# High and low part of a norm factor in different rows of one operand, spread by one matmul

## The chip, the cores and the metric

The kernel runs on one core of one Trainium2 chip. The metric is the device time of one execution in microseconds (us), lower is better.

## The reference

```python
kv  = einsum('bhsd,bhse->bhde', k, v)          # 8 batches, 8 heads, 576 tokens, 64 features
out = einsum('bhsd,bhde->bhse', q, kv)
rms = sqrt(mean(out * out, axis=-1, keepdims=True) + 1e-06)
x   = out / rms * g_norm                        # one factor 1/rms for each token and head
x   = x.transpose(0, 2, 1, 3).reshape(4608, 512)
x   = (sigmoid(x @ w_gate) * (x @ w_val)) @ w_mid      # 512 -> 1536 -> 512
h   = x @ w_in                                          # 512 -> 2048
out = where(h > 0, h, exp(min(h, 0)) - 1) @ w_out       # 2048 -> 512
```

All arrays are float32.

## The kernel before

Attention comes first (to about 178 us of the span), then the four large products, which take the rest. The large products use seven sub-products for each 2 by 2 block product, and split each operand into a high and a low part in a reduced float32 format (`F32R`), so that one product is three matmuls.

Attention works on pairs of heads: 8 batches of 4 pairs, 32 pairs in all. Each engine runs its own program, written out by hand, in the same numbered steps; only semaphores tie the engines together. In PE's step p (the code calls its place in a group of eight `r`):

- valid(0): six transposes of q of pair p (L825), then twelve matmuls k'v of pair p (L832), which wait until the kv copies of pair p-1 are out of PSUM
- valid(LO), LO = 1: q times kv of pair p-1, features in rows, tokens in columns, in two halves c = 0, 1 of 288 tokens (L841)
- valid(LB), LB = 7: "spread": the norm factors of pair p-7 are copied to the 64 feature rows of each head (L850 with the high part of the factor, L851 with the low part, for each half c), into PSUM `RB[c]`
- valid(LM), LM = 2: the sums of squares of pair p-2, again as high and low part, added into one PSUM bank `MS` over a whole batch of four pairs (L863, L865). For pair m and half c, head h, the sum lands in row 2(4c + m) + h, so 16 of the 128 rows hold something

After the last pair of a batch (steps with r = 1 or 5) ACT takes the root of all of `MS` (L1042, `rms`) and DVE takes the reciprocal (L1326, `rinv`). In the following step (r = 2 or 6) ACT rounds `rinv` to `r_hi` (L1026), and GpSimd (POOL) computes `r_lo = rinv - r_hi` (L794). PE's spread of the first pair of that batch stands in the step after (r = 3 or 7); it waits on `s_rlo` before its first matmul. I call the steps r = 1, 2, 3 (5, 6, 7) with this hand-over the batch boundary; it comes eight times, with the spreads of PE's steps 7, 11, 15, 19, 23, 27, 31 and 35.

The order on the other engines within a step is what this case turns on:

- DVE: copy kv of the step's pair from PSUM (L1310); `low_squares` for half 0 (L422); the two multiplies of `o` by the spread factor for pair p-7 (L1318); `copy_q` for two pairs ahead (L1301); in steps r = 1 and 5 the reciprocal (L1326)
- ACT: copies of the transposed q (L1019); in steps r = 2 and 6 `r_hi` (L1026); for each half `o` out of PSUM (L1034) and its square rounded (L1036); `copy_k` (L1009); in steps r = 1 and 5 `rms` (L1042)
- POOL: in steps r = 2 and 6 `r_lo` (L794); the squares of both halves (L802); `low_squares` for half 1 (L422)
- SP issues the loads of q, k, v three pairs ahead and the store of each finished pair

PE's spread of half c waits, beside `s_rlo`, for the multiply that read `RB[c]` last.

PE's steps from 32 on stand between the first sub-products of the gated product (L903); there DVE and ACT also split the first activations and form their sums (`sum_x`, L1358 to L1366), and POOL's `weight_sums` (L782 to L788) follows its last attention step. Constants are made by POOL at the start: `sum_f` holds 1/64 in the column of each head, `spread_f` a one in row 2n + h for the 64 columns of head h of factor row n; ACT and DVE wait for the count CONSTANTS.

Of the kernel before, what the change touches and what calls it, by code (L numbers as in the profile page):

```python
# [5 lines left out]
ALU = mybir.AluOpType  # L6
# [16 lines left out]
def build(  # L23
# [98 lines left out]
    with ctx:  # L122
# [23 lines left out]
        ident = ctx.enter_context(nc.sbuf_tensor("ident", [SP_, SP_], F32))  # L146

        with ExitStack() as stack:
            (qkv, sq, sq_hi, sq_lo, rinv, r_hi, r_lo, sum_w, spread_w, o, qt, kv, rms, raw_w, tmp_w, out_w, sum_f, spread_f,
             qk) = view(stack, [  # L150
                 ("qkv", [SP_, QR, 3, 2, RT, D], F32, 12 * KIB),
                 ("sq", [P, 2, HN], F32, 69 * KIB),
                 ("sq_hi", [P, 2, 2, HN], F32R, 69 * KIB + 2304),
                 ("sq_lo", [P, 2, 2, HN], F32R, 69 * KIB + 6912),
                 ("rinv", [P, HN], F32, 69 * KIB + 11520),
                 ("r_hi", [P, 2, HN], F32R, 69 * KIB + 12672),
                 ("r_lo", [P, 2, HN], F32R, 69 * KIB + 14976),
                 ("sum_w", [P, H, P + 2], F32R, 69 * KIB + 17280),
                 ("spread_w", [P, H, 2, D], F32R, 69 * KIB + 21440),
                 ("o", [P, RING, S], F32, buf_at(0)),  # L160
                 ("qt", [P, 2, S], F32, buf_at(0) + RING * S * 4),
                 ("kv", [P, 2, P], F32, buf_at(0) + (RING + 2) * S * 4),
                 ("rms", [P, HN], F32, buf_at(0) + (RING + 2) * S * 4 + KIB),
                 ("raw_w", [P, 2, 2048], F32, buf_at(1)),
                 ("tmp_w", [P, 2, 512], F32, buf_at(1) + 16 * KIB),
                 ("out_w", [P, 2, 2, 512], F32R, buf_at(1) + 20 * KIB),
                 ("sum_f", [P, H, P + 2], F32, buf_at(2)),
                 ("spread_f", [P, H, 2, D], F32, buf_at(2) + 4160),
                 ("qk", [SP_, QK, 2, RT, 2, D], F32, buf_at(3)),
             ])  # L170
# [257 lines left out]
        def ends_batch(r):  # L428
            return (r - LM) % NP == NP - 1
# [318 lines left out]
                sp.wait_ge(s_st[c], 16 * UNITS)  # L748


        IDENTITY, CONSTANTS = 2, 9

        @block.gpsimd
        def _(pool):
# [10 lines left out]
            pool.wait_ge(s_const, 6)  # L765

            for h in range(2):
                pool.memset(sum_f[h * D:(h + 1) * D, :, h:h + 1], 1.0 / D).then_inc(s_const, 1)
                pool.wait_ge(s_const, 7 + h)

            pool.affine_select(out=spread_f[:, :, :, :], in_=spread_f[:, :, :, :], compare_op=ALU.not_equal, fill=1.0,
                               base=0, pattern=[[-2, H], [-1, 2], [0, D]], channel_multiplier=1).then_inc(s_const, 1)
            pool.wait_ge(s_const, CONSTANTS)

            def weight_sums(c):

# [11 lines left out]
                pool.tensor_tensor(b21, b21, t2, ALU.subtract).then_inc(s_wsum, 1)  # L788

            def step(trip, r, valid):  # L790
                if valid(LM + 1) and ends_batch(r - 1):
                    b = batch_of(trip, r - LM - 1)
                    pool.wait_ge(s_rhi, b + 1)
                    pool.tensor_tensor(r_lo[:, batch_of(0, r - LM - 1) % 2, :], rinv[:, :], r_hi[:, batch_of(0, r - LM - 1) % 2, :].bitcast(F32),  # L794
                                       ALU.subtract).then_inc(s_rlo, 1)
                if valid(LO):
                    n = trip * RING + r - LO
                    for c in range(2):
                        pool.wait_ge(s_o_sb, 2 * n + c + 1)
                        wait_count(pool, s_sqlo[c], n)  # L800
                        src = o[:, (r - LO) % RING, half(c)]
                        pool.tensor_tensor(sq[:, c, :], src, src, ALU.mult).then_inc(s_sq, 1)  # L802
                    low_squares(pool, trip, r, 1)
# [10 lines left out]
        def _(pe):  # L814
            pe.wait_ge(s_const, IDENTITY)

            def step(trip, r, valid):
# [25 lines left out]
                if valid(LB):  # L843
                    n = p - LB
                    pe.wait_ge(s_rlo, batch_of(trip, r - LB) + 1)
                    for c in range(2):
                        wait_count(pe, s_x, 2 * n + c - 1)
                        w = spread_w[:, factor_rows(r - LB, c)].rearrange("p h d -> p (h d)")
                        b2 = batch_of(0, r - LB) % 2
                        pe.matmul(RB[c][:, 0:HN], w, r_hi[:, b2, :], start=True, stop=False)  # L850
                        pe.matmul(RB[c][:, 0:HN], w, r_lo[:, b2, :], start=False, stop=True).then_inc(s_rb, 1)  # L851
                if valid(LM):
                    n = p - LM
                    m = (r - LM) % NP
# [151 lines left out]
        def _(act):  # L1006
# [4 lines left out]
            def step(trip, r, valid, ahead=True):  # L1011
# [10 lines left out]
                if valid(LM + 1) and ends_batch(r - 1):  # L1022
                    b = batch_of(trip, r - LM - 1)
                    act.wait_ge(s_rinv, b + 1)
                    wait_count(act, s_rb, 2 * NP * (b - 1))
                    act.activation(r_hi[:, batch_of(0, r - LM - 1) % 2, :], rinv[:, :], ACT.Copy).then_inc(s_rhi, 1)  # L1026
                if valid(LO):
                    n = p - LO
                    if not isinstance(p, int) or n >= RING:
# [268 lines left out]
        def _(dve):  # L1298
# [4 lines left out]
            def step(trip, r, valid, ahead=True):  # L1303
# [15 lines left out]
                                                 op0=ALU.mult, op1=ALU.mult).then_inc(s_x, 1)  # L1319
                if ahead:  # L1320
                    copy_q(trip, r + LC)
                if valid(LM) and ends_batch(r):
                    b = batch_of(trip, r - LM)
                    dve.wait_ge(s_rms, b + 1)
# [282 lines left out]
```

## Time and profile before

| | |
|---|---|
| median of 3 runs | 1717.75 us (1716.82 to 1718.13) |
| profiled execution | 1718.92 us, its span 1716.8 us, 2.1 us outside the span |
| instructions | 27282 |
| TensorE matmul (PE) busy | 1652.0 us, 96% of the span |
| DVE, ACT, POOL busy | 1203.9 us, 839.5 us, 180.4 us |
| mean granted TensorE clock | 0.992 |
| chain that ended last | PE 72%, DVE 6%, ACT 5%, DMA 3% |

The span runs from the first to the last instruction. Matmuls are pipelined: the duration of one includes its way through the array, so what one more matmul costs in a row of them is the distance between starts, not the duration.

### The profile page before, as it was taken

What the parts mean: (1) busy time and instruction counts of PE and PEld (TensorE: products, weight loads), DVE (VectorE), ACT (ScalarE), POOL (GpSimd) and SP (SyncE); (2) the same over time, 40 slices, a digit from 0 to 9 for tenths busy, and PEclk for the clock granted to TensorE, in tenths of its full rate; (3) what the DMA queues carried; (4) which work ended last, traced back from release to release, by engine and by line L of the source; (5) the groups of instructions that cost most, each with busy time, mean ns of one, the idle gap of its engine ahead of it and who ended that gap; (6) DMA issues with size and microseconds to landing.
All of it is one profiled execution on the core that took longest, in us unless ns stands there. A gap on an engine that the chain in (4) does not pass through costs nothing.

```text
span 1716.8 us, 27282 instructions
## 1 busy us (share of the span) xinstructions
PE 1652.0 (96%) x10536; PEld 1628.6 (95%) x10536; DVE 1203.9 (70%) x1429; ACT 839.5 (49%) x1283; POOL 180.4 (11%) x185
## 2 busy tenths in 40 slices
PE   6998899999999999999999999999999799999999
PEld 5887899999999999999999989999999799999999
DVE  5778788887588755777777666776764667677664
ACT  6776455554455544444444444554453444444443
POOL 4555122221022100000000000000000000000000
PEclk9999899999999999999999999999999999999999
DMA  9885488887878645554444664323328833333341
GB/s 263 234 275 175 149 302 297 307 301 258 297 284 300 239 152 212 193 214 167 147 147 148 242 236 148 138 102 139 138 111 327 313 123 124 126 123 124 127 143 60
DMA packets 194745, 339.34 MB, mean 198 GB/s; under 512 B 13376, under 2 KB 149568, under 8 KB 194624
## 3 DMA queue, kind: packets, MB, share of 16 engines
q1 hardware_dynamic: 194624, 337.69, 56.2%
q8 instruction: 80, 1.31, 0.3%
q14 instruction: 41, 0.34, 0.1%
HBM read 191.89 MB, written 145.75 MB: 197 GB/s over the span
## 4 chain that ended last, share of the span: by engine, by line
PE 72%; DVE 6%; ACT 5%; issue 4%; DMA 3%; SPq 1%; POOL 0%; ACTq 0%; DVEq 0%; POOLq 0%
PE pair L903 36%; PE pair L968 21%; PE pair L936 15%; DVE s L1405 3%; DVE e L1510 2%; DMA u_elu<-s 1%; ACT e L1198 1%; DMA weight_items<-out_w 1%; DMA weight_items<-out_x 1%; ACT s L1217 1%; ACT e L1234 1%; ACT e L1229 1%; SPq L518 1%; DMA wreg<-weight_items 1%; ACT s L1208 0%
## 5 line engine op out<-in xcount | busy, mean ns | idle before, releaser
L903 PE MATMUL pair<-ring,wreg 128*128 128x384 f32 x5040 | 888.3, 336 | 29.5 <-ACT s L1217 15.3
L903 PEld LDWEIGHTS pair<-ring,wreg 128*128 128x128 f32 x5040 | 878.2, 189 | 38.5 <-ACT s L1217 20.7
L968 PE MATMUL pair<-wreg,ring 128*128 128x256 f32 x3024 | 364.9, 284 | 6.8 <-DMA wreg<-weight_items 6.8
L968 PEld LDWEIGHTS pair<-wreg,ring 128*128 128x128 f32 x3024 | 364.7, 193 | 7.0 <-DMA wreg<-weight_items 7.0
L1405 DVE TENSOR_TENSOR s<-s,pair 128x768 f32<-128x768 f32 (+1 forms) x252 | 210.5, 835 | 174.6 <-PE pair L903 139.4
L936 PE MATMUL pair<-ring,wreg 128*128 128x384 f32 x1512 | 262.2, 334 | 0.0
L936 PEld LDWEIGHTS pair<-ring,wreg 128*128 128x128 f32 x1512 | 262.1, 188 | 0.0
L1329 DVE TENSOR_TENSOR ring<-raw,ring 128x1024 fp32r<-128x1024 f32 (+1 forms) x162 | 180.7, 1133 | 112.5 <-ACT ring L1104 97.5
L1198 ACT ACTIVATE e<-e 128x768 f32<-128x768 f32 x72 | 61.0, 847 | 186.1 <-DVE e L1510 186.1
L1104 ACT ACTIVATE ring<-raw 128x1024 fp32r<-128x1024 f32 x108 | 111.8, 1051 | 55.9 <-DVE raw L1363 41.3
L1329 DVE TENSOR_TENSOR ring<-sum,ring 128x768 fp32r<-128x768 f32 (+1 forms) x90 | 91.8, 1031 | 30.3 <-ACT ring L1104 13.5
L1514 DVE SCALAR_TENSOR_TENSOR s<-e,s 128x768 f32<-128x768 f32 x72 | 69.0, 958 | 44.8 <-ACT e L1198 43.8
L1428 DVE TENSOR_TENSOR ub<-s 128x384 f32<-128x384 f32 x108 | 67.5, 625 | 12.4 <-ACT s L1125 5.3
L1329 DVE TENSOR_TENSOR ring<-x_raw,ring 128x768 fp32r<-128x768 f32 x72 | 72.0, 1003 | 0.7 <-ACT ring L1073 0.7
L1329 DVE TENSOR_TENSOR ring<-raw_k,ring 128x768 fp32r<-128x768 f32 x54 | 48.7, 953 | 22.6 <-ACT ring L1082 22.3
L1082 ACT ACTIVATE ring<-raw_k 128x768 fp32r<-128x768 f32 x54 | 41.8, 836 | 42.2 <-DVE raw_k L1363 22.6
L832 PE MATMUL pair<-qkv,qk 96*128 96x128 f32 x384 | 52.1, 288 | 2.9 <-DVE kv L1310 2.7
L832 PEld LDWEIGHTS pair<-qkv,qk 96*128 96x128 f32 x384 | 47.9, 200 | 4.4 <-issue 4.1
L1135 ACT ACTIVATE s<-s 128x384 f32<-128x384 f32 x36 | 19.0, 527 | 67.4 <-DVE s L1405 67.4
L1125 ACT ACTIVATE s<-s 128x384 f32<-128x384 f32 x36 | 19.0, 527 | 66.6 <-DVE s L1405 66.6
L1082 ACT ACTIVATE ring<-raw 128x768 fp32r<-128x768 f32 x54 | 41.6, 837 | 19.7 <-PE pair L936 19.7
L422 DVE TENSOR_TENSOR sq_lo<-sq,sq_hi 128x288 fp32r<-128x288 f32 x32 | 27.6, 861 | 30.3 <-POOL sq L802 28.3
(99 smaller groups left out, 1520.3 us busy)
## 6 DMA issues: line engine op xcount, KB each, us to landing
wreg<-weight_items SPq DMA_DIRECT2D x98, 512.0 KB, 6.4
raw<-u_elu SPq DMA_DIRECT2D x36, 1024.0 KB, 7.5
u_gated<-ub SPq DMA_DIRECT2D x144, 192.0 KB, 3.4
u_elu<-s SPq DMA_DIRECT2D x72, 384.0 KB, 2.4
weight_items<-out_w SPq DMA_DIRECT2D x50, 512.0 KB, 4.5
weight_items<-out_x SPq DMA_DIRECT2D x48, 512.0 KB, 4.5
x_raw<-x_attention SPq DMA_DIRECT2D x48, 384.0 KB, 5.5
raw_k<-u_gated SPq DMA_DIRECT2D x6, 2304.0 KB, 8.1
```

The source lines that it names most:

```text
L832: mm = pe.matmul(KV[:, 0:P], qk[:, r % QK, 1, t], qkv[:, r % QR, 2, :, t, :], start=(t == 0), stop=(t == RT - 1))
L903: mm = pe.matmul(dst[:, g, 0:NT], w[:, a, cols], ring[:, slot, b, kt, :], start=(i in STARTS and kt == a == b == 0), stop=(kt == 1 and a = ...
L936: mm = pe.matmul(dst[:, g, 0:NT], w[:, a, cols], ring[:, slot2(vis, i, t), b, kt, :], start=(i in STARTS and t == kt == a == b == 0), stop ...
L968: mm = pe.matmul(dst[:, 0, 0:256], s[:, b, 2 * c + kt, :], w[:, a, cols], start=(i in STARTS and c == kt == a == b == 0), stop=(c == 3 and ...
L1082: act.activation(ring[:, slot2(vis, i, t), 0], mid_item(i, t), ACT.Copy).then_inc(s_hi, 1)
L1104: act.activation(ring4[:, slot4(vis, i), 0], out_item(vis, i), ACT.Copy).then_inc(s_hi, 1)
L1198: act.activation(buf[:, :, :], buf[:, :, :], ACT.Exp).then_inc(s_exp, 1)
L1329: dve.tensor_tensor(dst, src, hi.bitcast(F32), ALU.subtract).then_inc(s_lo, 1)
L1405: dve.tensor_tensor(acc, acc, pp, ALU.add).then_inc(s_comb, 1)
L1428: dve.tensor_tensor(ub[:, m, :], acc[:, 1, :], acc[:, 0, :], ALU.mult).then_inc(s_u, 1)
L1510: dve.tensor_scalar(e[:, :, :], acc[:, :, :], 0.0, None, ALU.min).then_inc(s_min, 1)
L1514: dve.scalar_tensor_tensor(out=acc[:, :, :], in0=e[:, :, :], scalar=-1.0, in1=acc[:, :, :], op0=ALU.add, op1=ALU.max).then_inc(s_e, 1)
```

## The change

The factor's sums are made twice: `sum_f` gets a second column of 1/64 for each head, 64 columns further, so that rows 64 to 79 of `MS` (and of `rms` and `rinv`) repeat rows 0 to 15. `r_hi` and `r_lo` become one tile `r_parts`. ACT rounds all of `rinv` into it, and then rows 64 to 127 are overwritten by `rinv - r_parts`, the low part. `spread_f` gets a second set of ones, 64 rows further down, so that one matmul over 128 rows adds high and low part. The subtraction moves from POOL, where it was the first operation of its step, to DVE, where it stands behind `copy_q`, and has 64 rows instead of 128. POOL makes the constants with two more memsets and one more `affine_select`.

```diff
-                 ("r_hi", [P, 2, HN], F32R, 69 * KIB + 12672),
-                 ("r_lo", [P, 2, HN], F32R, 69 * KIB + 14976),
+                 ("r_parts", [P, 2, HN], F32R, 69 * KIB + 12672),
...
-        IDENTITY, CONSTANTS = 2, 9
+        IDENTITY, CONSTANTS = 2, 12
...
             for h in range(2):
-                pool.memset(sum_f[h * D:(h + 1) * D, :, h:h + 1], 1.0 / D).then_inc(s_const, 1)
-                pool.wait_ge(s_const, 7 + h)
-
-            pool.affine_select(out=spread_f[:, :, :, :], in_=spread_f[:, :, :, :], compare_op=ALU.not_equal, fill=1.0,
-                               base=0, pattern=[[-2, H], [-1, 2], [0, D]], channel_multiplier=1).then_inc(s_const, 1)
-            pool.wait_ge(s_const, CONSTANTS)
+                for at in (h, D + h):
+                    pool.memset(sum_f[h * D:(h + 1) * D, :, at:at + 1], 1.0 / D).then_inc(s_const, 1)
+            pool.wait_ge(s_const, 10)
+
+            for base in (0, -D):
+                pool.affine_select(out=spread_f[:, :, :, :], in_=spread_f[:, :, :, :], compare_op=ALU.not_equal,
+                                   fill=1.0, base=base, pattern=[[-2, H], [-1, 2], [0, D]],
+                                   channel_multiplier=1).then_inc(s_const, 1)
+                pool.wait_ge(s_const, 11 if base == 0 else CONSTANTS)
...
# POOL, step
-                if valid(LM + 1) and ends_batch(r - 1):
-                    b = batch_of(trip, r - LM - 1)
-                    pool.wait_ge(s_rhi, b + 1)
-                    pool.tensor_tensor(r_lo[:, batch_of(0, r - LM - 1) % 2, :], rinv[:, :], r_hi[:, batch_of(0, r - LM - 1) % 2, :].bitcast(F32),
-                                       ALU.subtract).then_inc(s_rlo, 1)
...
# PE, step, valid(LB)
-                        pe.matmul(RB[c][:, 0:HN], w, r_hi[:, b2, :], start=True, stop=False)
-                        pe.matmul(RB[c][:, 0:HN], w, r_lo[:, b2, :], start=False, stop=True).then_inc(s_rb, 1)
+                        pe.matmul(RB[c][:, 0:HN], w, r_parts[:, b2, :], start=True, stop=True).then_inc(s_rb, 1)
...
# ACT, step
-                    act.activation(r_hi[:, batch_of(0, r - LM - 1) % 2, :], rinv[:, :], ACT.Copy).then_inc(s_rhi, 1)
+                    act.activation(r_parts[:, batch_of(0, r - LM - 1) % 2, :], rinv[:, :], ACT.Copy).then_inc(s_rhi, 1)
...
# DVE, step
                 if ahead:
                     copy_q(trip, r + LC)
+                if valid(LM + 1) and ends_batch(r - 1):
+                    dve.wait_ge(s_rhi, batch_of(trip, r - LM - 1) + 1)
+                    low = r_parts[D:P, batch_of(0, r - LM - 1) % 2, :]
+                    dve.tensor_tensor(low, rinv[D:P, :], low.bitcast(F32), ALU.subtract).then_inc(s_rlo, 1)
                 if valid(LM) and ends_batch(r):
```

## Rows read from the trace of the kernel before

**Rows 1.** A stretch: length, busy PE, PEld, DVE, ACT, POOL; PE clock; DMA share, GB/s.

```profile
100.00:120.00 20.00, 19.39 (x148) 17.88 (x147) 15.50 (x33) 16.12 (x36) 12.14 (x16) 1.00 0.89 268
```

**Rows 2.** Groups by line, 0 to 260 us: busy us, mean ns, idle before.

```profile
L851 PE MATMUL pair<-r_lo,spread_w 128*128 128x288 f32 x64 | 18.6, 301 | 0.0
...
L794 POOL TENSOR_TENSOR r_lo<-rinv,r_hi 128x288 fp32r<-128x288 f32 x8 | 6.5, 808 | 30.1 <-ACT r_hi L1026 30.1
...
L771 POOL TENSOR_SCALAR_AFFINE_SELECT spread_f<-spread_f 128x1024 f32<-128x1024 f32 x1 | 1.2, 1167 | 0.1
```

**Rows 3.** Timeline of an ordinary step: start us, us, engine, line, operation.

```profile
85.75 0.66 PE L825 MATMUL pair<-ident,qk 96*128 96x96 f32 x6
...
88.38 0.51 PE L850 MATMUL pair<-r_hi,spread_w 128*128 128x288 f32 x1
...
88.72 0.29 PE L851 MATMUL pair<-r_lo,spread_w 128*128 128x288 f32 x1
...
89.64 0.66 PE L825 MATMUL pair<-ident,qk 96*128 96x96 f32 x6
```

**Rows 4.** Timeline of one batch boundary (PE's steps 21, 22, 23).

```profile
104.87 0.66 PE L825 MATMUL pair<-ident,qk 96*128 96x96 f32 x6
...
110.92 1.94 DVE L1326 RECIPROCAL rinv<-rms 128x288 f32<-128x288 f32 x1
...
112.79 0.41 DVE L1310 COPY kv<-pair 64x64 f32<-64x64 f32 x2
...
113.25 0.39 ACT L1034 ACTIVATE o<-pair 128x288 f32<-128x288 f32 x1
...
114.17 1.29 POOL L802 TENSOR_TENSOR sq<-o 128x288 f32<-128x288 f32 x2
...
114.76 1.14 PE L841 MATMUL pair<-qt,kv 128*128 128x288 f32 x4
114.87 0.91 DVE L422 TENSOR_TENSOR sq_lo<-sq,sq_hi 128x288 fp32r<-128x288 f32 x1 [1.67 <-POOL sq L802]
...
115.81 0.94 DVE L1318 SCALAR_TENSOR_TENSOR o<-o,g_col,pair 128x288 f32<-128x288 f32 x2
...
116.47 0.37 PE L850 MATMUL pair<-r_hi,spread_w 128*128 128x288 f32 x1 [0.58 <-DVE o L1318]
...
116.67 0.55 DVE L1301 COPY qk<-qkv 96x768 f32<-96x768 f32 x1
...
117.14 0.47 DVE L1310 COPY kv<-pair 64x64 f32<-64x64 f32 x2
...
117.71 0.66 PE L825 MATMUL pair<-ident,qk 96*128 96x96 f32 x6
```

**Rows 5.** Line 422 on DVE: ns min/median/max, first and last start.

```profile
L422 DVE TENSOR_TENSOR sq_lo<-sq,sq_hi x32: 479/903/918, 24.8 to 156.8; 128x288 fp32r<-128x288 f32 x32
```

**Rows 6.** Timeline at the first boundary (PE's step 7).

```profile
46.30 0.51 PE L850 MATMUL pair<-r_hi,spread_w 128*128 128x288 f32 x1
46.31 1.16 DVE L1301 COPY qk<-qkv 96x768 f32<-96x768 f32 x1
```

**Rows 7.** Timeline behind PE's step 31 (what PE waited for).

```profile
153.13 2.29 PE L841 MATMUL pair<-qt,kv 128*128 128x288 f32 x4 [1.79 <-DVE kv L1310]
```

**Rows 8.** The stretches before and behind it, columns as in the first group.

```profile
150.00:153.10 3.10, 1.34 (x8) 1.04 (x8) 3.01 (x5) 1.76 (x4) 2.97 (x3) 1.00 0.27 100
153.10:156.40 3.30, 3.27 (x9) 2.69 (x10) 3.26 (x5) 1.65 (x5) 1.59 (x3) 0.51 0.23 89
```

**Rows 9.** Timeline of the last boundary and what follows.

```profile
163.26 0.91 POOL L794 TENSOR_TENSOR r_lo<-rinv,r_hi 128x288 fp32r<-128x288 f32 x1 [4.92 <-ACT r_hi L1026]
...
169.10 4.21 PE L903 MATMUL pair<-ring,wreg 128*128 128x384 f32 x12 [4.09 <-ACT s L1122]
```

**Rows 10.** Line 1366, the sum S4 of the activations: ns min/median/max, first and last start.

```profile
L1366 DVE TENSOR_TENSOR sum<-x_raw,sum x18: 949/951/1950, 164.3 to 1245.1; 128x768 f32<-128x768 f32 x18
```

**Rows 11.** Waits between 45 and 145 us: total us, times, longest.

```profile
ACT qk L1009 <- DMA qkv<-in_k_dram: 7.3, 8, 3.1
```

More of the change, by code:

```diff
@@ L148, in build @@
         with ExitStack() as stack:
-            (qkv, sq, sq_hi, sq_lo, rinv, r_hi, r_lo, sum_w, spread_w, o, qt, kv, rms, raw_w, tmp_w, out_w, sum_f, spread_f,
+            (qkv, sq, sq_hi, sq_lo, rinv, r_parts, sum_w, spread_w, o, qt, kv, rms, raw_w, tmp_w, out_w, sum_f, spread_f,
              qk) = view(stack, [
```

## The prediction

> **What bounds the kernel now.** The change touches attention alone, a tenth of the span, so I read the table of stretches first: at 100 to 120 us PE is busy 19.39 of 20 us, at full clock [rows 1]. PE is the limit in an ordinary step. The groups by line give the size of the target: 64 low-part matmuls, 18.6 us busy [rows 2]. That is not what they cost. In the timeline of an ordinary step the starts run from 88.72 to 89.64 over seven matmuls, so one more costs 0.13 us [rows 3]. The step takes 89.64 - 85.75 = 3.89 us. All 64 would be worth 64 x 0.13 = 8.3 us if PE were the limit everywhere, half a per cent of the kernel.
>
> Then I followed one batch boundary through all engines, as the code's order says it must pass there through DVE [rows 4]. The reader is to see a chain that is not PE's: reciprocal at 110.92, kv copy behind it at 112.79, then PE's k'v matmuls, which need PSUM emptied by that copy, and q times kv at 114.76; and beside it ACT's `o` at 113.25, POOL's squares at 114.17, DVE's `low_squares` at 114.87, its multiplies at 115.81, and PE's spread at 116.47, for which PE stood idle 0.58 us. The reciprocal starts 110.92 - 104.87 = 6.05 us after the first of the three steps began, by way of that step's own `o`, squares and multiplies, and not by way of the spread matmuls. So in the three steps the end is set by DVE's order; only the fourth step of each batch is wholly PE's.
>
> **The change, part by part.**
>
> *Removed on PE.* Two of the four spread matmuls in each step: 0.26 us, so an ordinary step goes from 3.89 to 3.63 us. In the steps r = 1 and 2 this is taken back: PE reaches step r = 3 earlier by 0.52 us and waits that much longer for the kv copy, which still comes at 112.79. So q times kv stays at 114.76.
>
> *Removed on POOL.* `r_lo`, 0.81 us each [rows 2], stood ahead of the squares. Without it these start when `o` is there: 113.25 + 0.39 + 0.08 = 113.72 instead of 114.17, 0.45 us earlier. `low_squares` (114.42), the multiplies (115.36) and `copy_q` (116.22) follow 0.45 us earlier.
>
> *Moved to DVE.* The subtraction now stands behind `copy_q`, whose successor starts 117.14 - 116.67 = 0.47 us after it: 116.22 + 0.46 = 116.68. ACT's `r_hi` stands ahead of the `o` of 113.25 in ACT's order and is long done. PE's spread of this very step waits for the subtraction. What it lasts no row shows; the nearest is the same operation on 128 rows, with 288 elements in each: 0.48 at least, 0.90 median, 0.92 at most [rows 5]. Below 0.48 I see no reason, since what counts is the elements in a row, and halving the rows should do nothing. The long form is the one in which POOL's squares run beside it, and POOL's squares of the next step come up at about that time; I take 0.91 and keep 0.48.
>
> The Trainium skill has the same in "SBUF — State Buffer", section "Who interferes with whom": a VectorE instruction with two SBUF inputs and a GpSimd instruction that reads SBUF exclude each other, and the later one waits for the other's end. By it the subtraction takes 0.48 us or nearly twice that, according to who comes first, and the rows at 0.48 and 0.90 agree.
>
> *The sum at a boundary.* Spread at 116.68 + 0.91 + 0.10 = 117.69 instead of 116.47: +1.22. From there to the next step it took 117.71 - 116.47 = 1.24, of which 0.26 goes with the matmuls and some 0.10 was a wait for the second multiply, now past: 0.88. The next step starts at 118.57, +0.86. The fourth step gives back 0.26. A batch is longer by 0.60 us; with 0.48 for the subtraction by 0.17. What is queued behind the subtraction is the kv copy (117.14, now about 117.6), needed by PE only behind the transposes that start at 118.57, so nothing further is late. There are five such batches (spreads of steps 11 to 27): +3.0 us (0.85 to 3.2).
>
> *First boundary.* Spread at 46.30, without a wait, while `copy_q` starts at 46.31 and takes 1.16 [rows 6]. Now `copy_q` at 45.86, the subtraction behind it at about 47.0 and alone on the port, 0.48, spread at 47.5: +1.2, less 0.4 as above: +0.8.
>
> *Spread of step 31.* There is no `copy_q` any more; the subtraction comes before the first activation sums and the kv copy for which PE waits until 153.13 [rows 7]: about 0.75 us more on DVE less 0.45 from POOL, +0.3, less 0.26 from step 28: +0.05.
>
> *The tail.* After 153.13 PE runs without a wait to the last sums of squares, first at half clock (0.51 [rows 8], so a matmul costs 0.26): two removed at 0.26, two at 0.13: -0.8. Then comes DVE: reciprocal, multiplies, now the subtraction (+0.5), then sum S4, on which ACT's queue and PE's start at 169.10 hang [rows 9]. S4 is the first of its 18 and took 1.95 against 0.95 for the median [rows 10], while POOL ran `weight_sums`, held back to 164.1 by its wait of 4.92 us for `r_hi` [rows 9]. Without that wait POOL is through before S4. That would give back 1.0, but puts POOL beside earlier DVE work; I take -0.3 in all (+0.5 to -0.5). The spread of step 35 lies in PE's wait of 4.09 and gives nothing. The four matmuls removed in steps 36 and 37 lie on the path to the next DVE result: 0.5 to 0.8, taken as -0.6.
>
> *Nothing.* The second `affine_select` (1.17 us [rows 2]) and two small memsets at the start lie under the first loads, for which POOL's weight sums and ACT's and DVE's first copies wait; uncovered they would cost some 1.3 us once. `MS`, `rms`, `rinv` keep their shapes.
>
> Sum: +0.8 + 3.0 + 0.05 - 0.8 - 0.3 - 0.6 = +2.2 us. On the profiled execution that is 1718.9 + 2.2 = 1721.1 us, its span 1719.0; it stands 1.2 above the median of the runs, so for the median 1717.75 + 2.2 = 1720.0 us.
>
> **The rivals.**
>
> *The plain gain (faster).* The subtraction is hidden and all removed matmuls count: -8.3 us, some more at half clock, 1709. It would need the subtraction done when PE could first use it: after two steps of 3.63 and 88.38 - 85.75 = 2.63 of the third [rows 3], 104.87 + 7.26 + 2.63 = 114.76, which is two microseconds before DVE even starts it; and the kv copy out of the way. Against it stands the whole chain of [rows 4]; for it only that I may have misread an order. 0.08.
>
> *The clock falls at the boundaries (slower).* PE's idle time before the spread grows from 0.58 to 0.58 + 1.22 = 1.80 us. After a wait of 1.79 us the clock was granted at half for 3.3 us [rows 7, 8], which costs half of that, 1.65 us. In six batches this is up to 9.9 us (1730), in half of them 5 (1725). The wait of 0.58 [rows 4] left it at full [rows 1]. Against it: before 153.13 PE was busy 1.34 of 3.10 us [rows 8], while here q times kv and the k'v matmuls run right up to the gap. It decides as soon as the gap is enough by itself. 0.17. The Trainium skill ("TensorE: Matmul & The Clock Gate", section "What's actually happening") says that half clock is the resting state and activity lifts it, which leaves both open.
>
> *Loads get room (faster, but little).* ACT waits 8 times for k, 7.3 us, once 3.1 [rows 11], with DMA busy 0.89 [rows 1]. The loads, issued by PE's progress, get a longer batch for the same bytes. If the longest wait goes, -3.1: 1717; with the short subtraction 1714.5. Against it: PE's ordinary steps ask for more bytes a microsecond than before. 0.15.
>
> **How the numbers follow.** The forecast, the stall that eats the gain, has 0.60 and a range of its own of 1717.5 to 1721.5. What can be told from no change is 0.2%, 3.4 us: 1714.3 to 1721.2. Faster: the plain gain 0.08 and a third of the loads 0.05, 0.13. Slower: the clock 0.15 and the upper edge of the forecast 0.08, 0.23. The same: 0.64. The range reaches from the loads with the short subtraction (1714.8) to half the boundaries at half clock (1726); the plain gain and more falls of the clock are left out.
>
> **What would show it.** Right: PE's distance between step starts 3.63 in ordinary steps; the three boundary steps together 13.7 instead of 12.84; PE's spread waiting about 1.8 us for DVE's subtraction on the boundary, which lasts 0.9; POOL's squares at the end of `o`; S4 near 0.95. Wrong: the subtraction at 0.3 us or less; PE's wait still on the multiplies; half clock between 60 and 150 us; ordinary steps still at 3.89, because ACT, which is busy 16.1 of 20 us, or DMA takes over.

## The result and the profile after

The changed kernel takes 1721.17 us (16 runs, 1717.29 to 1725.28), the kernel before 1717.56 us on the same chip (16 runs): ratio 1.0024, interval 1.0015 to 1.0032. Timed once more (e7_changed_again) it took 1718.75 against 1716.93 us, ratio 1.0014 (1.0005 to 1.0023). It is slower by 0.14 to 0.24%, about as much as can just be told from no change; the forecast was 1720.0 with 1714.8 to 1726.0. The profiled execution took 1720.49 us, its span 1718.7 (before: 1716.8), its mean granted clock 0.987 (before: 0.992).

The page of the changed kernel: span, and busy time of each engine.

```profile
span 1718.7 us, 27154 instructions
...
PE 1651.2 (96%) x10472; PEld 1629.0 (95%) x10472; DVE 1203.5 (70%) x1437; ACT 840.7 (49%) x1283; POOL 173.4 (10%) x180
```

128 instructions are gone and PE's busy time is 0.8 us less, yet the span is 1.9 us longer.

The timeline of the same boundary as in [rows 4], PE's steps 21, 22 and 23 (line numbers are smaller by 4):

```profile
103.53 0.66 PE L822 MATMUL pair<-ident,qk 96*128 96x96 f32 x6
...
107.17 0.66 PE L822 MATMUL pair<-ident,qk 96*128 96x96 f32 x6
...
109.60 1.94 DVE L1326 RECIPROCAL rinv<-rms 128x288 f32<-128x288 f32 x1
...
111.46 0.41 DVE L1306 COPY kv<-pair 64x64 f32<-64x64 f32 x2
...
112.02 1.58 PE L829 MATMUL pair<-qkv,qk 96*128 96x128 f32 x12 [0.55 <-DVE kv L1306]
112.39 1.29 POOL L799 TENSOR_TENSOR sq<-o 128x288 f32<-128x288 f32 x2 [3.49 <-ACT o L1030]
113.09 0.90 DVE L421 TENSOR_TENSOR sq_lo<-sq,sq_hi 128x288 fp32r<-128x288 f32 x1 [1.22 <-POOL sq L799]
...
114.88 0.55 DVE L1297 COPY qk<-qkv 96x768 f32<-96x768 f32 x1
115.34 1.51 POOL L799 TENSOR_TENSOR sq<-o 128x288 f32<-128x288 f32 x2 [0.69 <-ACT o L1030]
115.46 0.86 DVE L1321 TENSOR_TENSOR r_parts<-rinv,r_parts 64x288 fp32r<-64x288 f32 x1
...
116.37 0.54 PE L847 MATMUL pair<-r_parts,spread_w 128*128 128x288 f32 x2 [1.81 <-DVE r_parts L1321]
...
117.27 0.66 PE L822 MATMUL pair<-ident,qk 96*128 96x96 f32 x6
...
120.91 0.66 PE L822 MATMUL pair<-ident,qk 96*128 96x96 f32 x6
```

Read the distances. An ordinary step is 107.17 - 103.53 = 3.64 us, before 3.89. The three boundary steps together are 117.27 - 103.53 = 13.74 us, before 12.84. PE meets the kv copy early and waits for it 0.55 us. The squares start 0.47 us after `o` (111.92) instead of 0.92 us, `low_squares` follow, but then the spread waits 1.81 us for the subtraction, where it waited 0.58. The batch of four steps is 17.38 us, before 16.74.

Seven steps further on is the one ordinary step that differs, PE's step 28. Its timeline, and behind it a stretch of it (columns as in [rows 1]):

```profile
134.73 0.66 PE L822 MATMUL pair<-ident,qk 96*128 96x96 f32 x6
135.22 2.74 PE L829 MATMUL pair<-qkv,qk 96*128 96x128 f32 x12
...
140.01 0.66 PE L822 MATMUL pair<-ident,qk 96*128 96x96 f32 x6
```

```profile
137.00:140.00 3.00, 3.00 (x15) 2.61 (x15) 0.44 (x2) 1.01 (x4) 0.53 (x1) 0.71 1.07 328
```

This step takes 5.28 us without any wait. The twelve k'v matmuls take 2.74 us instead of 1.53: the granted clock is 0.71 in the stretch, so it went from 1.2 to 2.4 GHz within it, and 5.28 - 3.64 = 1.64 us is what that cost.

Stretch by stretch, by the starts of PE's steps (us):

| stretch | before | after | |
|---|---|---|---|
| start to step 7 | 42.25 | 40.89 | -1.36, not the change: the thirteen profiles have 40.5 to 42.6 here, whatever the edit |
| step 7 (first boundary) | 5.36 | 6.73 | +1.37 |
| steps 8 to 27, five batches | 86.84 | 87.11 | +0.27 |
| steps 28 to 30 | 11.68 | 12.55 | +0.87: one step at half clock +1.64, less 3 x 0.26 |
| step 31 to the large products | 36.27 | 36.71 | +0.44 |
| the rest | 1534.4 | 1534.7 | +0.3 |

The line of the five batches needs its parts. Before they took 16.80, 17.46, 19.10, 16.74 and 16.74 us: the second and third contain the waits for k [rows 11]. After they took 17.47, 17.38, 17.44, 17.36 and 17.46, and no wait for a load is left between 45 and 145 us. So the chain costs 5 x 0.67 = +3.3 us, and 3.1 us of load waits have gone under it. Which batches such waits stretch differs from profile to profile (below); the chain is in every one.

### The profile page after: what moved, and what is told of

It is laid out like the page before. It is cut to its first block, busy times and chain, and to the rows that moved or that the text cites. A ratio compares the mean times of both kernels' runs of the same rounds, so it can differ in the third digit from the quotient of the medians.

```text
span 1718.7 us, 27154 instructions
## 1 busy us (share of the span) xinstructions
PE 1651.2 (96%) x10472; PEld 1629.0 (95%) x10472; DVE 1203.5 (70%) x1437; ACT 840.7 (49%) x1283; POOL 173.4 (10%) x180
## 4 chain that ended last, share of the span: by engine, by line
PE 74%; DVE 6%; ACT 4%; issue 3%; DMA 2%; SPq 1%; POOL 0%; ACTq 0%; DVEq 0%; POOLq 0%
PE pair L899 38%; PE pair L964 21%; PE pair L932 15%; DVE s L1405 3%; DVE e L1510 2%; DMA u_elu<-s 1%; ACT e L1194 1%; ACT s L1213 1%; ACT e L1230 1%; ACT e L1225 1%; DMA wreg<-weight_items 1%; DMA weight_items<-out_x 0%; ACT s L1204 0%; ACT ring L1090 0%; DVE ring L1329 0%
## 5 line engine op out<-in xcount | busy, mean ns | idle before, releaser
L1329 DVE TENSOR_TENSOR ring<-raw,ring 128x1024 fp32r<-128x1024 f32 (+1 forms) x162 | 180.7, 1134 | 112.9 <-ACT ring L1100 97.8
L1329 DVE TENSOR_TENSOR ring<-sum,ring 128x768 fp32r<-128x768 f32 (+1 forms) x90 | 92.3, 1037 | 30.2 <-ACT ring L1100 13.5
L1329 DVE TENSOR_TENSOR ring<-x_raw,ring 128x768 fp32r<-128x768 f32 x72 | 75.9, 1056 | 0.7 <-ACT ring L1069 0.7
L1428 DVE TENSOR_TENSOR ub<-s 128x384 f32<-128x384 f32 x108 | 61.0, 564 | 12.4 <-ACT s L1121 5.3
L1329 DVE TENSOR_TENSOR ring<-raw_k,ring 128x768 fp32r<-128x768 f32 x54 | 48.7, 954 | 22.6 <-ACT ring L1078 22.3
L799 POOL TENSOR_TENSOR sq<-o 128x288 f32<-128x288 f32 x64 | 45.0, 723 | 64.0 <-ACT o L1030 64.0
```

The source lines that it names most:

```text
L1329: dve.tensor_tensor(dst, src, hi.bitcast(F32), ALU.subtract).then_inc(s_lo, 1)
L1428: dve.tensor_tensor(ub[:, m, :], acc[:, 1, :], acc[:, 0, :], ALU.mult).then_inc(s_u, 1)
```

## The experiments

A "batch" is below the distance of four step starts; the value is the one of undisturbed batches. Before, it is 16.74, after 17.4.

**Low part on POOL again (e1_low_on_pool).** The merged operand stays, the subtraction goes back to where it was:

```diff
             def step(trip, r, valid):
+                if valid(LM + 1) and ends_batch(r - 1):
+                    pool.wait_ge(s_rhi, batch_of(trip, r - LM - 1) + 1)
...
+                    pool.tensor_tensor(low, rinv[D:P, :], low.bitcast(F32), ALU.subtract).then_inc(s_rlo, 1)
+                    pool.wait_ge(s_rlo, batch_of(trip, r - LM - 1) + 1)
```

> The merged matmul with the subtraction (64 rows) back on POOL, first in its step; POOL waits for its own previous operation before it and for the subtraction itself after it. By the theory of the chain (DVE's order sets the batch boundary, and the subtraction behind copy_q is what costs) the spread of the boundary starts where it did before, behind the multiplies, PE saves 0.26 us there and 0.26 in the fourth step: a batch of 16.2 us instead of 16.7, some 3 us in attention and 1 to 1.5 in the tail, 4.5 below the kernel before: 1713. PE's wait ahead of the spread about 0.6 us. By the rival that the clock alone made the changed kernel slower, the same, as the wait is short again. By the rival that loads hold attention, the time stays at that of the kernel before, within 1 us.

1715.00 us, ratio 0.9986 (0.9977 to 0.9996); batches 16.80, 18.07, 16.99, 16.77, 16.71. The loss is gone, but the expected 1713 is missed by 2 us, and the undisturbed batch is that of before, not 16.2: what is gained on the kernel before lies outside of it. POOL in the boundary step that begins at 102.69:

```profile
111.32 0.79 POOL L798 TENSOR_TENSOR r_parts<-rinv,r_parts 64x288 fp32r<-64x288 f32 x1 [3.27 <-ACT r_parts L1029]
112.34 1.29 POOL L806 TENSOR_TENSOR sq<-o 128x288 f32<-128x288 f32 x2 [0.23 <-POOL r_parts L798]
```

Half the rows take POOL as long as all (0.79 against 0.81), and the wait for its own result, which this edit added, costs 0.23 us more. `low_squares` starts 10.35 us after the first of the three steps, before 10.00, after 9.56. What PE saves in the fourth step is lost again here.

**Low part on DVE, early (e2_low_early, e11_low_early_again).** In the changed kernel the three lines of the subtraction move up from behind `copy_q` to behind the kv copies, ahead of `low_squares`:

```diff
                         dve.tensor_copy(kv[rows, r % 2, rows], KV[rows, rows]).then_inc(s_kv_sb, 1)
+                if valid(LM + 1) and ends_batch(r - 1):
+                    dve.wait_ge(s_rhi, batch_of(trip, r - LM - 1) + 1)
+                    low = r_parts[D:P, batch_of(0, r - LM - 1) % 2, :]
+                    dve.tensor_tensor(low, rinv[D:P, :], low.bitcast(F32), ALU.subtract).then_inc(s_rlo, 1)
                 if valid(LO):
                     low_squares(dve, trip, r, 0)
```

> The changed kernel with DVE's subtraction moved up, from behind copy_q to right behind the kv copies of the same step, where DVE waited 1.2 to 1.7 us for POOL's squares. By the theory of the chain the subtraction costs nothing there, POOL's squares keep their gain of 0.45 us, the spread waits only for the multiplies, and a batch takes 15.8 us against 16.7 before and 17.4 in the changed kernel: about 8 us below the kernel before, 1709.5, and 11 below the changed one. If loads become the limit (4.7 MB a batch ask for 300 GB/s) a batch stays at 16.2 or more and the time above 1712. If the place of the subtraction did not matter, it would stay at 1721.

1708.65 us, ratio 0.9953 (0.9935 to 0.9972); batches 15.88, 16.85, 16.22, 16.67, 15.93. The timeline at the same boundary:

```profile
107.58 0.41 DVE L1306 COPY kv<-pair 64x64 f32<-64x64 f32 x2
...
108.18 0.46 DVE L1310 TENSOR_TENSOR r_parts<-rinv,r_parts 64x288 fp32r<-64x288 f32 x1 [0.18 <-ACT r_parts L1022]
...
109.22 0.90 DVE L421 TENSOR_TENSOR sq_lo<-sq,sq_hi 128x288 fp32r<-128x288 f32 x1 [0.58 <-POOL sq L799]
...
110.81 0.73 PE L847 MATMUL pair<-r_parts,spread_w 128*128 128x288 f32 x2
```

The subtraction fits into the time in which DVE waits for the squares anyway, and DVE still waits 0.58 us behind it. PE's spread has no wait. Where batches are longer than 15.9, ACT waits for k:

```profile
ACT qk L1005 <- DMA qkv<-in_k_dram: 6.9, 10, 1.6
```

Run again on another chip:

> The changed kernel with the subtraction right behind the kv copies, once more, for its interval: 1708 to 1710, ratio 0.995 to 0.9965 to the kernel before, and batches of 15.9 us where no load is waited for.

1708.39 us, ratio 0.9945 (0.9928 to 0.9962); batches 15.90, 16.79, 16.25, 16.21, 16.38. So the merged operand and the early subtraction together gain half a per cent on the kernel before; e5 below tells what each of them is worth.

**The move alone (e3_move_alone).** The kernel before, with two matmuls for each half, but the subtraction (all 128 rows) on DVE behind `copy_q`:

```diff
-                    pool.tensor_tensor(r_lo[:, batch_of(0, r - LM - 1) % 2, :], rinv[:, :], r_hi[:, batch_of(0, r - LM - 1) % 2, :].bitcast(F32),
...
                     copy_q(trip, r + LC)
+                if valid(LM + 1) and ends_batch(r - 1):
...
+                    dve.tensor_tensor(r_lo[:, batch_of(0, r - LM - 1) % 2, :], rinv[:, :], r_hi[:, batch_of(0, r - LM - 1) % 2, :].bitcast(F32),
+                                       ALU.subtract).then_inc(s_rlo, 1)
```

> The kernel before with one part of the change: r_lo (128 rows) computed by DVE behind copy_q instead of by POOL; both spread matmuls stay. By the theory of the chain the spread of a boundary starts 1.2 us later and nothing is given back by PE: 1.1 us more in each of six batches, 1.2 at the first boundary, little in the tail: 8 us above the kernel before, 1725.5, more if the clock falls. By the rival that the move is hidden and something else made the changed kernel slower: 1717.5.

1719.41 us, ratio 1.0014 (1.0004 to 1.0024); batches 17.36 to 17.46. The expectation of 1725.5 was missed: the move makes the boundary longer, but the subtraction lasts half as long as I had taken.

```profile
116.47 0.55 DVE L1296 COPY qk<-qkv 96x768 f32<-96x768 f32 x1
...
116.93 0.98 POOL L797 TENSOR_TENSOR sq<-o 128x288 f32<-128x288 f32 x1 [0.69 <-ACT o L1029]
116.94 0.45 DVE L1320 TENSOR_TENSOR r_lo<-rinv,r_hi 128x288 fp32r<-128x288 f32 x1
...
117.44 0.40 PE L845 MATMUL pair<-r_hi,spread_w 128*128 128x288 f32 x1 [1.29 <-DVE r_lo L1320]
```

With 128 rows it takes 0.45 us, in the changed kernel with 64 rows 0.86. The batch is as long as that of the changed kernel: 0.41 us less of subtraction pays for the removed matmuls that count. What makes the difference in the subtraction is the question of e9 and e10.

**Two matmuls, early (e5_early_two_matmuls).** The same lines behind the kv copies:

> The kernel before with r_lo (128 rows) computed by DVE right behind the kv copies, both spread matmuls kept: the other half of the early placement. By the theory of the chain a boundary ends 0.45 us earlier than before (POOL's squares start at the end of o) and the ordinary step stays at 3.89: a batch of 16.3 us, 1715, against 15.9 and 1708.6 for the early placement with the merged matmul. So with the subtraction out of the way the merged matmul is worth 5 to 6 us, while behind copy_q it was worth -2. By the rival that the early placement alone made the gain: 1709 to 1710.

1713.17 us, ratio 0.9983 (0.9974 to 0.9992); undisturbed batches 16.29 and 16.37. In the early place the merged matmul is worth 4.5 us against e2, a little less than the 5 to 6 expected. This completes a table of place and form (median us, undisturbed batch us):

| low part | two matmuls | one matmul, merged |
|---|---|---|
| on POOL | before: 1717.4, 16.74 | e1: 1715.0, 16.75 |
| on DVE, behind `copy_q` | e3: 1719.4, 17.4 | after: 1721.2 and 1718.8, 17.4 |
| on DVE, behind the kv copies | e5: 1713.2, 16.29 | e2, e11: 1708.7 and 1708.4, 15.89 |

The middle row does not compare like with like: e3 subtracts 128 rows in 0.45 us, the changed kernel 64 rows in 0.86. The pairs that do are in a second table, behind e10.

**Why 0.86 (e9_all_rows_in_place, e10_64_rows_own_tile).** e9 is the changed kernel with the subtraction over all 128 rows, in place:

```diff
-                    low = r_parts[D:P, batch_of(0, r - LM - 1) % 2, :]
-                    dve.tensor_tensor(low, rinv[D:P, :], low.bitcast(F32), ALU.subtract).then_inc(s_rlo, 1)
+                    low = r_parts[:, batch_of(0, r - LM - 1) % 2, :]
+                    dve.tensor_tensor(low, rinv[:, :], low.bitcast(F32), ALU.subtract).then_inc(s_rlo, 1)
```

> The changed kernel with the subtraction over all 128 rows of r_parts, still in place and behind copy_q. It leaves the high part out of the spread factor (rows 0 to 63 are overwritten too), the work of every engine is otherwise the same. Tells whether the 64 rows make the subtraction take 0.86 us where the 128 rows of r_lo took 0.45. If it is the rows, it takes 0.45 here, the batch is 17.0 us and the time some 2 us below the changed kernel; if it is the operation in place, it still takes 0.86, 17.4 us, and the same time.

1715.07 us, ratio 0.9986 (0.9974 to 0.9998); batches 16.83 to 16.93, and 17.26 once. The timeline:

```profile
115.42 0.55 DVE L1297 COPY qk<-qkv 96x768 f32<-96x768 f32 x1
...
115.88 0.98 POOL L799 TENSOR_TENSOR sq<-o 128x288 f32<-128x288 f32 x1 [0.69 <-ACT o L1030]
115.89 0.45 DVE L1321 TENSOR_TENSOR r_parts<-rinv,r_parts 128x288 fp32r<-128x288 f32 x1
```

e10 is e3 with the subtraction over rows 64 to 127 only, out of place, `r_lo` cleared once at the start:

```diff
-                    dve.tensor_tensor(r_lo[:, batch_of(0, r - LM - 1) % 2, :], rinv[:, :], r_hi[:, batch_of(0, r - LM - 1) % 2, :].bitcast(F32),
+                    dve.tensor_tensor(r_lo[D:P, batch_of(0, r - LM - 1) % 2, :], rinv[D:P, :], r_hi[D:P, batch_of(0, r - LM - 1) % 2, :].bitcast(F32),
```

> The kernel with the move alone (two spread matmuls, r_lo behind copy_q), with the subtraction on rows 64 to 127 only and its own output tile. It leaves the low part out of the factor (the rows that the spread reads are set to zero at the start). If the 64 rows are the cause, it takes 0.86 here, the batch is 17.9 us and the time 1722 or more; if the operation in place is, 0.45, 17.4 us and 1719.5.

1725.76 us, ratio 1.0054 (1.0034 to 1.0074). Its profile is of the slowest of its five runs, and each of the five batches has steps at half clock; the boundary steps free of it take 6.22 to 6.33 us, which with three ordinary steps makes a batch of 17.9. The two groups by line, ns min, median and max, of e9 and of e10:

```profile
L1321 DVE TENSOR_TENSOR r_parts<-rinv,r_parts x8: 442/448/821, 47.3 to 164.7; 128x288 fp32r<-128x288 f32 x8
```

```profile
L1321 DVE TENSOR_TENSOR r_lo<-rinv,r_hi x8: 455/864/872, 46.4 to 179.6; 64x288 fp32r<-64x288 f32 x8
```

So it is neither the tile nor working in place, but the rows: 64 to 127 against all 128. The starts tell how. On 128 rows the subtraction starts 0.47 us behind the start of the copy, which lasts 0.55 (e3 and e9), level with POOL's squares to 0.02 us, and POOL's multiply then takes 0.98 us for one half. On rows 64 to 127 it starts 0.58 us behind the copy's start, when that copy has ended; POOL's squares start 0.12 us earlier (115.34 and 115.46 above), and DVE is the one that waits. The Trainium skill, "SBUF — State Buffer", section "Who interferes with whom", says that of the two the one that issues first has the shared read port for its whole instruction and the other is fully blocked. The trace agrees as to who waits: second in line, the subtraction takes 0.86 - 0.45 = 0.41 us more, and POOL's multiply 0.98 us instead of 0.66. Each loses some 0.14 us less than the other's record still lasts.

Why the start is later, the traces tell in part, and it is not the number of rows. The first kv copy has 64 rows too, but rows 0 to 63, and behind the same `copy_q` it starts 0.47 us after its start (116.67 and 117.14 in [rows 4]). The second kv copy, on rows 64 to 127, starts 0.03 us after the first has ended, 32 times of 32 in the kernel before; and the subtraction on rows 64 to 127 starts 0.03 us after the end of `copy_q` at all 25 batch boundaries of the five profiles that have it there. So in these traces a DVE operation that starts at row 64 waits for the end of one that starts at row 0. That this makes the difference for the subtraction is not tested by itself: a kernel with the low part in rows 0 to 63 was not run.

With e3, e9, e10 and e6 (below), the late place splits as follows (undisturbed batch us, median us):

| subtraction behind `copy_q` | two matmuls | one matmul, merged |
|---|---|---|
| 128 rows, 0.45 us | e3: 17.4, 1719.4 | e9: 16.9, 1715.1 |
| rows 64 to 127, 0.86 us | e10, e6: 17.9, 1725.8 and 1727.3 | after: 17.4, 1721.2 and 1718.8 |

The merged matmul saves 0.5 us a batch in both rows, here too, and the 64-row form costs 0.5 us a batch in both columns. The changed kernel is slower because of what the late place (0.66, before to e3) and the 64-row form (0.5) cost together, not because the removed matmuls give nothing.

**The same matmul twice, and the changed kernel again (e6_same_matmul_twice, e7_changed_again).** e6 is the changed kernel with each spread matmul issued twice:

```diff
+                        pe.matmul(RB[c][:, 0:HN], w, r_parts[:, b2, :], start=True, stop=True)
                         pe.matmul(RB[c][:, 0:HN], w, r_parts[:, b2, :], start=True, stop=True).then_inc(s_rb, 1)
```

> The changed kernel with its spread matmul issued twice for each half (the second writes the same values again), so that PE has as many matmuls as before and DVE, ACT and POOL run the changed kernel's programs. Tells why the subtraction takes 0.86 us in the changed kernel and 0.45 in the kernel with the move alone. If it is PE's earlier step starts that shift DVE against POOL, it takes 0.45 here, a batch is 17.4 and the time 1719.5 as with the move alone. If it is the form of the operation (64 rows, or in place), it still takes 0.86 here, a batch is 17.9 us and the time 1723 or more.

> The changed kernel once more, on the same chip as its variants: 1721, mean granted clock 0.988 against 0.9915 of the kernel before in the same call. The kernel with the filler matmuls had 0.991 and 1719.5; if the clock explains that difference this run shows the lower clock again together with a time 1.5 to 2 us above it; if the difference was one of chips, it has 1719.5 here.

e6: 1727.28 us, ratio 1.0069 (1.0056 to 1.0083), undisturbed batches 17.89 to 18.00. e7: 1718.75 us, ratio 1.0014, batches 17.37 to 17.48 and one of 19.12. The doubled matmuls cost 17.9 - 17.4 = 0.5 us in a batch, four at 0.13 and not eight: 0.26 in the fourth step and 0.26 behind the late spread; those of the steps r = 1 and 2 vanish in the wait for kv, as the forecast had it. e7 was expected at 1721 and came out 2 us faster, at the lower clock (0.9892) all the same. Two of e6's batches took 19.6, each with one step at half clock, straight behind a boundary's wait:

```profile
82.69 0.40 PE L847 MATMUL pair<-r_parts,spread_w 128*128 128x288 f32 x1 [1.82 <-DVE r_parts L1322]
...
83.86 0.92 PE L822 MATMUL pair<-ident,qk 96*128 96x96 f32 x6
84.57 2.82 PE L829 MATMUL pair<-qkv,qk 96*128 96x128 f32 x12
...
89.39 0.66 PE L822 MATMUL pair<-ident,qk 96*128 96x96 f32 x6
```

That step takes 5.53 us. The eight short matmuls behind the wait run at 2.4 GHz (0.13 us apart), and the clock falls only with the step behind them, as it does in step 28 of the changed kernel.

**Filling the wait (e4_filler).** The changed kernel with ten matmuls of no use in PE's wait, at seven boundaries. They write with the start flag into unused columns of the bank in which the sums of squares accumulate, and the norm factors are not the reference's; the work is the same.

```diff
+                    if (r - LB) % NP == 0 and not (isinstance(p, int) and p >= PAIRS):
+                        for _ in range(FILL):
+                            pe.matmul(MS[:, HN:512], spread_w[:, 0:1].rearrange("p h c d -> p (h c d)"),
+                                      sum_w[:, :, :].rearrange("p n c -> p (n c)")[:, 0:512 - HN], start=True, stop=True, skip_group_check=True)
                     pe.wait_ge(s_rlo, batch_of(trip, r - LB) + 1)
```

> The changed kernel with ten matmuls of 128 x 224 without use, put ahead of PE's wait for the subtraction at seven of the eight boundaries (output to unused columns of the bank of the sums of squares), some 0.9 us of work inside a wait of 1.8. They delay nothing, so the distances of the steps stay (a batch of 17.4 us). By the theory that the clock's falls make up what the forecast missed (2 us in the median, 8 us of spread between runs of the changed kernel), the granted clock rises from 0.987 to 0.990 or more, the spread between runs shrinks, and the median is 1718.5 to 1719.5. If the clock has no part in it, the median stays at 1721.

1719.5 us, ratio 1.0014 (1.0004 to 1.0024). At a boundary:

```profile
116.58 1.49 PE L845 MATMUL pair<-sum_w,spread_w 128*128 128x224 f32 x10
...
118.84 0.53 PE L852 MATMUL pair<-r_parts,spread_w 128*128 128x288 f32 x2 [0.77 <-DVE r_parts L1326]
```

The wait is 0.77 us instead of 1.81. No step of the five batches is at half clock in this profile, and the runs' clock is 0.9912 on average, as before (0.9916), against 0.9878 and 0.9892 of the changed kernel. In time it decides nothing: the fillers cost some 0.06 us in each batch and 1.1 us at the first boundary, where they ran at half clock, and the ratio is that of e7. The spread between the runs was expected to shrink and did not: it is 8 us (1714.3 to 1722.3) as in the changed kernel.

**The kv copy ahead of the reciprocal (e8_kv_copy_first).** From e2, the reciprocal moves behind the next step's kv copies, for which PE waits:

```diff
                 if valid(LM + 1) and ends_batch(r - 1):
+                    b = batch_of(trip, r - LM - 1)
+                    dve.wait_ge(s_rms, b + 1)
...
+                    dve.reciprocal(rinv[:, :], rms[:, :]).then_inc(s_rinv, 1)
```

> The kernel with the early subtraction and, beside it, DVE's reciprocal moved behind the kv copies of the following step (order: kv copy, reciprocal, subtraction, low_squares, multiplies). Tests the step of the forecast that PE reaches the third step early and then waits for the kv copy behind the reciprocal. By the chain PE's wait of 0.55 us ahead of the k'v matmuls goes, the later links come 0.4 us later and the spread may wait for the multiplies instead: a batch of 15.4 to 15.9 us, 1706 to 1709. If loads are the limit by now (batches of 15.9 to 16.9 with the early subtraction), nothing changes: 1708 to 1709.

1711.33 us, ratio 0.9965 (0.9951 to 0.9979); batches 16.39 to 16.50 and 17.29. Slower than e2, and missed:

```profile
110.58 1.26 PE L838 MATMUL pair<-qt,kv 128*128 128x288 f32 x4 [0.34 <-ACT sq_hi L1032]
112.51 0.74 PE L847 MATMUL pair<-r_parts,spread_w 128*128 128x288 f32 x2 [0.67 <-DVE o L1323]
```

The wait for kv is gone (it was 0.82 us here), but ACT rounds `r_parts` as its first work of that step and waits for the reciprocal; `o` and its square come later, PE waits for them (0.34), and DVE's multiplies are late for the spread (0.67).

## Why the forecast held, and where it did not

- *Ordinary step 3.89 to 3.63.* Shown: 3.63 to 3.64.
- *The boundary is set by DVE's order, and the gain of steps r = 1 and 2 is taken back by the kv copy.* Shown by three pairs of runs that differ in the number of spread matmuls while the subtraction is equally long and in the same place: e3 to e9 and e6 to after with the low part late, e5 to e2 with it early. Each is worth 0.4 to 0.5 us a batch, where the eight matmuls removed would make 1.04; the rest comes back as PE's wait for kv (0.55 us in the changed kernel, none in e6).
- *The sum at a boundary, +0.60 for a batch.* Measured +0.62 to +0.73, the three steps 13.74 for 13.7, the spread's wait 1.81 to 1.90 for 1.80. With the short subtraction the forecast had +0.17, and e9 has 16.83 to 16.93, +0.09 to +0.19.
- *The subtraction at 0.91.* Measured 0.86 in the five batches, and 0.45 to 0.46 only where POOL wasn't beside it. But the reason that I gave had a hole: "halving the rows should do nothing". Taking rows 64 to 127 makes the operation start 0.11 us later, and thereby lose the port to POOL. With 128 rows it takes 0.45, the lower bound, and the time is below that of the kernel before (e9, 1715.07, which leaves out the high part). The value was right because the squares did come first; my own times for both (116.68 for the subtraction, and squares "at about that time") could not tell which.
- *First boundary +0.8.* The whole of step 7 is +1.37. The subtraction took 0.45 as said and ended at 46.14, but the profile shows no wait of PE for it: k'v at 42.79 and q times kv behind it ran at half clock (granted 0.50 from 43.25 to 46.5), and the spread started only at 46.61. At full clock PE would have been there at 44.96 and have waited until about 46.24 (an estimate from these starts), so half clock adds some 0.4 us to a wait that would have come anyway.

```profile
42.79 2.57 PE L829 MATMUL pair<-qkv,qk 96*128 96x128 f32 x12 [0.99 <-DVE kv L1306]
```

It does so in all seven profiles with the subtraction behind `copy_q` (after, e3, e4, e6, e7, e9, e10) and in none of the other six, although PE's waits ahead of it are the same in both (0.43 and 1.0 us). What lowers it there is open.
- *The clock falls at the boundaries, 0.17.* Partly true: one step of 1.64 us in each profile of the changed kernel, two in e6, more in e10, none in e2, e5 or e11. Counted over the batch boundaries (steps 11 to 27) of all profiles: behind waits of 1.81 to 1.91 us the clock fell at 8 of 20 (one of 5 in after and in e7, two in e6, four in e10), behind waits of up to 1.4 us at none of 45. So the long wait belongs to it, but what picks the one boundary and not the next is open. The mean clock of an execution is no measure of it: in the profile after, PE was at half clock for 7 us near 990 us, in the large products, and before not at all; in e1, whose waits are short, for 7 us too. Nor does it explain the spread of the runs. Those of the changed kernel at a clock of 0.985 took 1724.3 to 1725.3 us, those at 0.990 took 1717.3 to 1718.9, but the kernel before spreads as widely (1714.0 to 1726.1) at 0.990 to 0.994.
- *Loads get room, 0.15.* True in the profile: 3.1 us of k waits went with the longer batches. In the sum this rival and the clock's (+1.64) stand against the chain's +3.3.
- *Spread of step 31, +0.05.* From step 28 to the end of the wait for kv it was 19.97 us instead of 18.68, of which 1.64 is the step at half clock: -0.35.
- *The tail, -0.8, -0.3 and -0.6.* This step failed as a whole: from the end of that wait (153.13 and 154.70) to the large products +0.02 instead of -1.7. The timeline of the changed kernel:

```profile
154.70 1.24 PE L838 MATMUL pair<-qt,kv 128*128 128x288 f32 x4 [1.66 <-DVE kv L1306]
...
159.77 1.28 POOL L784 TENSOR_TENSOR tmp_w<-raw_w 128x512 f32<-128x512 f32 x1
159.93 1.94 DVE L1329 TENSOR_TENSOR ring<-sum,ring 128x768 fp32r<-128x768 f32 x1
...
161.02 0.50 ACT L1038 ACTIVATE rms<-pair,eps_col 128x288 f32<-128x288 f32 x1 [3.43 <-PE pair L861]
161.79 0.93 DVE L1314 SCALAR_TENSOR_TENSOR o<-o,g_col,pair 128x288 f32<-128x288 f32 x2
...
162.64 1.94 DVE L1326 RECIPROCAL rinv<-rms 128x288 f32<-128x288 f32 x1
...
166.26 0.46 DVE L1321 TENSOR_TENSOR r_parts<-rinv,r_parts 64x288 fp32r<-64x288 f32 x1
166.75 0.96 DVE L1366 TENSOR_TENSOR sum<-x_raw,sum 128x768 f32<-128x768 f32 x1
```

and that of the kernel before, where `rms` starts at 160.22:

```profile
158.44 0.95 DVE L1329 TENSOR_TENSOR ring<-sum,ring 128x768 fp32r<-128x768 f32 x1
...
160.75 1.95 DVE L1326 RECIPROCAL rinv<-rms 128x288 f32<-128x288 f32 x1 [0.39 <-ACT rms L1042]
```

PE's part came in number only: from the end of its wait to `rms` 6.32 us instead of 7.09. I had reckoned with half clock as before; but here it was granted in full, q times kv took 1.24 us instead of 2.29; behind it the first sub-product and a wait of 0.28 us for DVE's multiplies took 0.5 us more than before. That -0.8 was met is luck. S4 came as said: 0.96 instead of 1.95. But POOL, no longer held, begins its weight sums at 159.77, 0.16 us ahead of the remainder on L1329, which takes 1.94 us instead of 0.95. The multiplies behind it end late, and the reciprocal starts 1.62 us after `rms` instead of 0.53: +1.1, which with the subtraction's +0.6 is more than S4 gave back. I had named this ("puts POOL beside earlier DVE work"), but -0.3 in all leaves only 0.2 us for it. From `rms` to PE's start behind S4 it is +0.7. Steps 36 and 37, taken as -0.6, gave +0.1: from PE's start behind S4 on the distance is 13.41 instead of 13.30 us. The first two matmuls removed there save 0.29 us, but PE stays at half clock for 5.6 us instead of 4.5, and the second sub-product takes 2.64 us instead of 2.11; the other two lie ahead of a wait of 0.56 us for DVE.

So the time was met by a sum with a right main term (+3.0, measured +3.3) and misses that cancel: tail +1.7, the step at half clock +1.6, first boundary +0.6, the rest +0.3; against them loads -3.1, step 31 -0.4, and a start earlier by 1.4 that has nothing to do with the change. The main term is borne out by e2, e3, e5, e6 and e9; that the total fits so closely is luck.

## What to carry to other kernels

Removed matmuls are worth what is left of them behind the waits for other engines: here 0.4 to 0.5 of 1.04 us a batch, wherever the subtraction stood. The small operation that moves along with such a change can cost more than that. Behind a copy, and on rows 64 to 127, it turned the saving into a loss; in a place where its engine waited anyway the same change gains half a per cent. Before fixing the cost of an operation with two SBUF inputs, compare its start with that of the neighbour on POOL to a tenth of a microsecond, since the later one waits for the other; and a wait that is taken from POOL lets its next work run into another part of DVE's queue. A wait on PE that grows to nearly two microseconds costs, beyond itself, now and then a step at half clock.

## What the runs showed of the hardware that was not expected

- The same DVE subtraction takes 0.45 us on 128 rows and 0.86 on rows 64 to 127 (e3, e9 against after, e6, e7, e10). The latter starts 0.58 instead of 0.47 us behind the start of a copy that begins at row 0, and so comes second at the port that it shares with POOL. A copy of rows 0 to 63 behind the same copy starts at 0.47.
- Between subtraction and squares that start within 0.02 us of each other POOL was the one that waited, ten times of ten (e3, e9), also where its record starts first.
- POOL takes 0.79 us for 64 rows (e1) and for 128 (before, median), and waiting for its own result costs it 0.23 us.
- In the batches half clock came only behind waits of 1.8 to 1.9 us, at 8 of 20 such boundaries, and PE had then been busy again for 1.3 to 1.7 us (read in short stretches once each in after, e6, e7 and e10). At the first boundary it came behind a wait of 1.0 us, 0.3 to 0.4 us after PE had started again (after, e3, e7).
